# Second routing made per step of the first expert layer, in a fused attention and two-layer mixture-of-experts kernel

## The reference

```python
# layer 1: one expert a row
logits = x @ w_gate + modality_bias[modality_id]
e_idx  = argmax(logits); gate_w = softmax(logits)[e_idx]
out[mask] = gate_w * (relu(x[mask] @ w1[e]) @ w2[e])
# layer 2: two experts a row, routed by the output of layer 1
noisy = x @ w_gate + log1p(exp(x @ w_noise)) * noise
top2, top2_w = the two largest of noisy, softmax over them
out[mask] += top2_w[k] * (relu(x[mask] @ w1[e]) @ w2[e])
```

## Time and profile before

| | |
|---|---|
| median of 3 runs | 987.11 us (986.29 to 988.6) |
| the profiled execution's own time | 985.47 us |
| its span, first to last instruction | 983.7 us |
| mean granted TensorE clock | 0.967 |
| PE busy | 906.2 us, 92% |
| DVE busy | 540.5 us, 55% |
| ACT busy | 230.3 us, 23% |
| POOL busy | 349.9 us, 36% |

### The profile page before, as it was taken

How to read it: one execution, slowest core, us unless ns; L and a number is a source line. 1 busy time by engine, 2 the same in 40 slices (tenths; PEclk the granted TensorE clock), 3 DMA queues, 4 the chain that set the end, 5 groups by cost and what they waited for, 6 DMA issues and landing times.

```text
span 983.7 us, 22470 instructions
## 1 busy us (share of the span) xinstructions
PE 906.2 (92%) x7285; PEld 876.3 (89%) x7286; DVE 540.5 (55%) x968; ACT 230.3 (23%) x435; POOL 349.9 (36%) x364
## 2 busy tenths in 40 slices
PE   5999999999999999591499999999999999999995
PEld 5888887999999999591399999999999999999995
DVE  8888999784333343257663544435435454443532
ACT  2232333112011121054221222203213131221210
POOL 7333334324221313101542433423443424334232
PEclk9999999999999999895699999999999999999998
DMA  6676782219111112253253534525334443522233
GB/s 250 193 229 228 257 289 92 65 44 390 50 50 33 56 40 57 69 178 119 50 186 73 122 103 112 110 36 127 96 56 104 115 109 108 116 33 52 47 48 50
DMA packets 54594, 111.69 MB, mean 114 GB/s; under 512 B 8704, under 2 KB 35712, under 8 KB 54528
## 3 DMA queue, kind: packets, MB, share of 16 engines
q1 hardware_dynamic: 34896, 71.27, 21.7%
q0 software_dynamic: 15744, 34.70, 17.3%
q10 hardware_dynamic: 3888, 4.89, 1.4%
HBM read 84.84 MB, written 26.00 MB: 113 GB/s over the span
## 4 chain that ended last, share of the span: by engine, by line
PE 82%; DVE 12%; issue 3%; DMA 1%; DVEq 1%; ACT 1%; POOL 0%; POOLq 0%
PE ps L1660 22%; PE ps L1662 21%; PE ps L1661 21%; PE ps L1570 3%; PE ps L1530 2%; PE ps L1534 2%; PE ps L1476 2%; DVE grow L898 2%; PE ps L1499 2%; PE ps L1561 1%; DVE scores L913 1%; PE ps L1585 1%; PE ps L1597 1%; PE ps L1524 1%; DVE rest L883 1%
## 5 line engine op out<-in xcount | busy, mean ns | idle before, releaser
L1660 PE MATMUL ps<-x_hi,weights 128*128 128x256 f32 x984 | 279.1, 284 | 4.6 <-DVE x_lo L1374 2.6
L1662 PE MATMUL ps<-x_hi,weights 128*128 128x256 f32 x984 | 278.5, 283 | 0.0
L1661 PE MATMUL ps<-x_lo,weights 128*128 128x256 f32 x984 | 278.2, 283 | 0.0
L829 ACT ACTIVATE hid_hi<-ps 128x512 fp32r<-128x512 f32 x164 | 98.0, 598 | 539.7 <-PE ps L1662 533.1
L1379 DVE SCALAR_TENSOR_TENSOR hid_lo<-ps,hid_hi 128x512 fp32r<-128x512 f32 x164 | 112.8, 690 | 194.2 <-ACT hid_hi L829 172.5
L1660 PE MATMUL ps<-weights,hid_hi 128*128 (+1 forms) x616 | 214.2, 348 | 1.2 <-DVE hid_lo L1379 1.2
L1662 PE MATMUL ps<-weights,hid_lo 128*128 (+1 forms) x616 | 207.3, 336 | 0.0
L1661 PE MATMUL ps<-weights,hid_hi 128*128 (+1 forms) x616 | 207.2, 336 | 0.0
L1660 PEld LDWEIGHTS ps<-x_hi,weights 128*128 128x128 f32 x984 | 187.4, 190 | 6.6 <-issue 6.5
L1661 PEld LDWEIGHTS ps<-x_lo,weights 128*128 128x128 f32 x984 | 187.4, 190 | 0.0
L1662 PEld LDWEIGHTS ps<-x_hi,weights 128*128 128x128 f32 x984 | 187.2, 190 | 0.0
(11 more groups left out here) (281 smaller groups left out, 1064.4 us busy)
## 6 DMA issues: line engine op xcount, KB each, us to landing
stage<-in_moe_w_dram SPq DMA_DIRECT2D x18, 1536.0 KB, 8.2
kv_in<-in_kv_T_dram SPq DMA_DIRECT2D x24, 512.0 KB, 5.7
kv_in<-in_kv_T_dram SPq DMA_DIRECT2D x24, 448.0 KB, 3.4
w_in<-in_w_T_dram SPq DMA_DIRECT2D x24, 258.5 KB, 4.2
out_dram<-zeros SPq DMA_DIRECT2D x26, 192.0 KB
x_rows<-y_tok ACTq DMA_DIRECT2D x24, 192.0 KB
stage<-moe_rows SPq DMA_DIRECT2D x12, 384.0 KB, 4.2
stage<-in_moe_w_dram SPq DMA_DIRECT2D x2, 768.0 KB, 7.7
```

What stands on the lines that cost most here:

```text
L829: act.activation(hid_hi[:, 2 * q:2 * q + 2, :], h_ps[q], ACT.Relu).then_inc(s_hhi[l], 1)
L1660: pe.matmul(out_ps, hi, by_hi, start=first, stop=False)
L1661: pe.matmul(out_ps, hi, by_lo, start=False, stop=False)
L1662: return pe.matmul(out_ps, lo, by_hi, start=False, stop=final)
```

## The change

The pass between the layers is taken out. Instead:

- **Extra columns.** For each expert of layer 1 in use, PE multiplies the transposed w2 (a new input, loaded by SP with `load_w2T`) by layer 2's gate and noise weights (`expert_columns`, 24 f32 products with 16 columns); ACT and DVE split the result (`split_v`, `low_v`) into 16 columns beside w2. Down products of layer 1 are 400 wide; their last 16 columns are the row's second logits before its gate weight.
- **Row chains.** Two steps after step s, its rows are routed (`row_logits`, `row_first`, `row_second`, `row_places` on DVE; Exp, Ln, Exp on ACT; two small products on PE, `row_ranks`). DVE does the first two ahead of `hidden_low(s, 0)`. Noise and gate weight come in a row of `nz_dram`, gathered by POOL (`gather_noise`); SP writes the gate part once, after `first_gates`, which DVE does at the start of step 2.
- **Lists.** Each row's two entries (row number and weight) go to per-expert lists in DRAM, by four indirect writes of 8 bytes a row (`list_rows` on POOL).
- **Change of layers.** At step 11 POOL reads what the lists hold of expert 0 (of the first nine steps) and gathers the rows of layer 2's first two steps (`early_slots`). The rows of steps 11 and 12 are routed at the end of step 11, in step 12 and in layer 2's step 0. There DVE also makes the second layer's tables (`second_tables`). SP reads all lists back once.
- **Weights** of both layers are one array and one order of loading. moe_rows is cleared during attention, `out` right after it.

Cut to its core (order of each engine's new work):

```diff
@@ SP, start and each attention chunk
+            sp.dma_start(nz_dram[:, 0:E], noise).then_inc(s_noise, 16)
+            sp.wait_ge(s_const, 5)
+            sp.dma_start(list_dram..., list_sb[:, :, :]).then_inc(s_fill, 16)
...
+                clear_row(g)
+                if late(b, c) == 6:
+                    load_w2T(lookup(sp, first_i, 0, E - 1))
@@ SP, after attention
+            for g in range(G + TS):
+                clear(g)
+            sp.wait_ge(s_gate1, 1)
+            sp.dma_start(nz_dram[:, E:2 * E]..., gate_two[:, :, :]).then_inc(s_noise, 16)
...
+            with sp.Fori(1, E) as n:
+                with sp.If(n < runs):
+                    sp.wait_ge(s_vmm, n)
+                    load_w2T(lookup(sp, run_expert, n, E - 1))
+                    load_run(n, lookup(sp, run_expert, n, E - 1))
@@ POOL, first_layer_step
+                    if peeled and s == ONE:
+                        early_slots()
...
+                    split_next(s)
+                    rows_read(s + 2)
+                    gather(s + 3, 1 - u)
+                    if peeled and s == 2:
+                        pool.wait_ge(s_noise, 32)
+                        gather_noise(0, 0, early_src)
+                        gather_noise(1, 1, early_src)
+                    elif peeled and s == 3:
+                        list_rows(1)
+                        gather_noise(2, 0, early_src)
+                        list_rows(2)
+                        gather_noise(3, 1, src_row)
+                    elif late:
+                        list_rows(s)
+                        gather_noise(s, 2, src_row)
+                    elif not peeled or s > 3:
+                        list_rows(s - LAG + 1)
+                        gather_noise(s, 2 if peeled and s == ONE else u, src_row)
+                    scatter(s, j, u)
+                    if peeled and s == ONE:
+                        list_rows(ONE)
@@ POOL, early_slots
+                pool.wait_ge(s_listed, CUT * 2 * TS * 16)
+                # waits for the scatters of steps 0 to 10
+                pool.dma_start(early_list...).then_inc(s_earlylist, 16)
+                ...four gathers to first_rows_in, and a wait for them
@@ DVE, first_layer_step (row = (number, buffer, landed, ...) of step s - 2)
+                    if peeled and s == 2:
+                        first_gates()
+                    if peeled and s == 3:
+                        row_places(1, 0, early_src[:, 0:TS], None)
+                    if row:
+                        row_logits(...)   # waits for the noise of the row
+                        row_first(...)    # waits for ACT's Exp and Ln
                     hidden_low(s, 0)
+                    if row:
+                        row_second(row[0])
...
+                        if row:
+                            row_places(...)
+                        with dve.If(lookup(dve, v_now, s, 1) > 0):
+                            low_v(run + 1, v_ps)
...
                         split_x(s + 1, 1 - u, 1)
...
+                    if peeled and s == 2:
+                        row_logits(1, 0, 32, early_dst[:, 0:TS])
+                    if peeled and s == ONE:
+                        row_logits(ONE, ...); row_first(ONE, 0); row_second(ONE)
                     result_copy(...)
+                    if peeled and s == 2:
+                        row_first(1, 0); row_second(1)
+                    if peeled and s == ONE:
+                        row_places(ONE, ...)
@@ PE, slot_step
                     up(s, 0, run)
+                    if l == 0 and peeled and s == 3:
+                        row_ranks(1)
...
+                        with pe.If(lookup(pe, v_now, s, 1) > 0):
+                            expert_columns(..., v_ps)   # waits for load_w2T
+                    if l == 0 and late:
+                        row_ranks(s)
+                    elif l == 0 and (not peeled or s > 2):
+                        row_ranks(s - LAG + 1)          # waits for row_second
+                    elif l == 1 and peeled and s == 0:
+                        row_ranks(rows_done)
                     down_second(s, 0, run, two)
```

More of the change, by code:

```diff
@@ L96, in attention_moe_moe @@
                   small[:, at[2]:at[3]].rearrange("p (c e) -> p c e", e=2 * E)]
-        noise_sb = small[:, at[3]:at[4]].rearrange("p (g e) -> p g e", e=E)
-        with ExitStack() as early:
-            y_tok = [early.enter_context(nc.sbuf_tensor(f"y_tok{i}", [P, C], F32)) for i in range(2)]
-            with nc.sbuf_tensor("block_ones", [P, P], F32) as block_ones:
-                pass
-            sx, sy = ([early.enter_context(nc.sbuf_tensor(f"{n}0", [P, TS, CX], F32))] for n in ("sx", "sy"))
@@ L106, in attention_moe_moe @@
-        gx_hi = [sb(f"gx_hi{i}", [P, CC, P], F32R) for i in range(NGT)]
-        gx_lo = [sb(f"gx_lo{i}", [P, CC, P], F32R) for i in range(NGT)]
-        sb("gap", [P, 16])
-        gate_split = sb("gate_split", [P, CC, 4 * E], F32R)
-        both = sb("both", [4 * E, 2 * E])
+        WSZ = CC * F
+        y_tok = [sb(f"y_tok{i}", [P, C]) for i in range(2)]
+        with nc.sbuf_tensor("block_ones", [P, P], F32) as block_ones:
+            pass
+        sx, sy = [sb(f"sx{i}", [P, TS, C]) for i in range(2)], [sb("sy0", [P, TS, C])]
@@ L1425, in slot_step @@
                             with dve.If(change > 0):
-                                low_w1(l, run + 1, q)
+                                low_w1(run + 1, q)
+                        if row:
+                            row_places(row[0], row[1], row[4], row[5], peeled and s == ONE)
+                        with dve.If(lookup(dve, v_now, s, 1) > 0):
+                            low_v(run + 1, v_ps)
+                            dve.wait_ge(s_vlo, run + 2)
+                            dve.nop(nofuse=True)
+                        split_x(s + 1, 1 - u, 1)
+                        with dve.If(fresh > 0):
+                            low_w2(run + 1)
                     else:
@@ L1652, in early @@
+                    last.then_inc(s_code, 1)
                 def early(s):
```

1217 lines of the change are left out of this document (675 added, 542 removed).

## The result

The changed kernel takes 1045.72 us (median of four runs, 1043.63 to 1049.42), beside it the kernel before 986.7 (984.55 to 988.6): ratio 1.060, 95% interval 1.056 to 1.065. It is slower, as forecast, but by 59 us where 24 were forecast, and 1045.7 lies outside the range.

What follows compares the result with a forecast made beforehand. Both layers were taken as bound by TensorE's own matmuls, the second routing pass as a hole. Profiled 985.5 + 3 attention + 15.4 lateness + 6 clock = 1009.9, forecast 1010 us, slower; range 958 to 1040.

Steps and rivals of the forecast that it cites:

- four waits out of five: Five long TensorE waits forecast, of 10, 9, 9, 7 and 17 us.
- steps 5 to 9: Layer one: POOL keeps up, DVE's row chain makes each step 19.0 us, 1.4 more each, 7.0 in all.
- Step 2: Layer one: TensorE waits 10 us for the second run's transposed w2; the step takes 15.5 us more.
- columns 4.9: Layer one, 24 f32 products with 16 columns at 0.2 us each: 4.9 us on the path.
- one sum of 6: Clock term: 6 us in all for running at the 1.2 GHz level after the long waits.
- Steps 3 and 4: Layer one: late noise behind POOL's work, then DVE's row chains; step 3 takes 14.3 us more, step 4 9.4.
- Rival 2: POOL becomes the bound, list writes 1.9 us instead of 1.3, noise late in steps 4 to 11: 1030 us, chance 0.14.
- Step 10: Layer one's weight change: DVE's weight parts, row_places and splits hold TensorE; 21.2 us for 13.9, 7.3 more.
- Step 11: Layer one, two rows: TensorE waits in row_ranks(11) until 24.4, product at 24.7; the step takes 7.1 us more.
- Step 12 to layer two: Largest wait, noise behind early_slots: layer two's first product 40.3 us after step 12's start, before 97.9; 57.6 less.
- some 30 operations: DVE's second_tables with the list read make layer two's second step 3.5 us longer.
- The gap's gain: Between the layers: removing the routing pass saves 80.3 us; step 12's start to layer two took 97.9 before.

Runs made afterwards that it cites:

- w2T_first: Changed kernel with the second run's transposed w2 loaded before SyncE waits for the gate weights: 1026.4 us, ratio 1.039 to the kernel before.
- noise_first: Changed kernel with GpSimd's noise gathers moved ahead in step 2, first row's list writes and third noise gather ahead in step 3: 1022.8 us, ratio 1.035.
- best1: Changed kernel with noise_first, early_last and w2T_first edits, row chain later, early slots directly behind step 11's scatter, second_tables cut in two: 1000.2 us, ratio 1.011.
- before_writes: Kernel before with four indirect 8-byte-piece writes added to each layer-one step, read by nothing: 1027.1 us (1.039) on chip C; repeated on chip A, 993.9 (1.005).
- best1_no_lists: best1 without the list writes, so layer two works on padding rows: 979.8 us, ratio 0.990 to the kernel before.
- best2: best1 with list writes held until the first transposes of the step's middle, noise gathers behind the token gather: 985.2 us (0.997), again 981.3 (0.992).
- early_last: Changed kernel with early slots' preparation behind step 11's scatter and list writes, its noise gather ahead of all: 1032.4 us, ratio 1.043.

## Why the prediction was wrong

The side was right, the mechanism right for four waits out of five, the size wrong. The step that failed most is the account of steps 5 to 9: the list writes' effect on TensorE stood at nothing, and the row chain at 1.4 us a step; the runs show some 10 us of late completions there and 2.2 to 2.6 a step. Behind it come the columns' clock (4.9 forecast, 10.4 measured) and second_tables. Point by point:

- **Step 2, and the columns.** The wait was 8.35 (forecast 10), ended by the transposed w2's landing, as forecast. The term "columns 4.9" was mis-sized: 10.4, at clock 0.50. I had charged the clock loss to the waits in one sum of 6; here it is 5.5 for the columns and 2.1 for the down products behind them. w2T_first shows that the wait is only part of the reason: without it the columns still took 7.8. In step 0 the columns took 5.4 and then the first 14 of the 48 down products ran at half level: 11.0 in all instead of 8.65. The up products there took 1.95 more, with a wait of 2.12 for first_counts in them that I had not priced.
- **Steps 3 and 4.** Together 28.6 for 23.7. The wait in row_ranks(1) is there (9.70, at 280.51; I had the product at 260 to 268.8, with the noise in 11 us earlier: DVE got it at 275.08, since GpSimd stood 7.71 for transposes that came late with step 2, which ran 5.8 over its forecast). What I placed as a wait for noise in step 4 was a wait for the list in step 3: row_places(2) may not overwrite its entries before list_rows(1) has landed, and that is issued only at 302.83, behind the gather that waits for the middle of step 3. I had read the wait on s_listed in the diff and not run it through GpSimd's order. noise_first takes both out at once: 16 us less; it does not part them.
- **Steps 5 to 9**, the largest miss, 14.3 of the 37 us. "POOL keeps up" held. The chain's price of 1.4 a step was low: on chip A, without late completions, these steps take 19.8 to 20.1 on average, 2.2 to 2.6 more than 17.6. The other 10 or so in this execution (some 20 on chips B and C) go with completions of TensorE that come late while GpSimd sends the list writes: the prediction charged these writes only to GpSimd's own time, and put their effect on TensorE at nothing. No term or rival had it. The trace of before shows it in small, and at no cost. In its step 2, with four indirect transfers just issued, ACT starts the second quarter's half 1.15 us behind its last product instead of 0.32, and 0.41 to 0.53 in steps 4 to 9:

```profile
220.92 0.28 PE L1662 MATMUL ps<-x_hi,weights 128*128 128x256 f32 x1
...
222.07 0.60 ACT L829 ACTIVATE hid_hi<-ps 128x512 fp32r<-128x512 f32 x1 [2.36 <-PE ps L1662]
```

  Rival 2 forecast a time near the measured one (1030, by a full GpSimd), for a reason that did not happen: GpSimd is busy 63.8 of 130 us. Without these 10 us the kernel would take near 1036 (an estimate, 1045.7 less 10): inside the range, still at twice the change forecast, and that would have been luck.
- **Step 10**: 7.2 for 7.3, and by the way forecast: DVE's split of x behind row_places ends the wait at 21.4 (21.2 forecast). On chip A it is 6.5.
- **Step 11**: 10.1 for 7.1. The product of row_ranks(11) comes at 25.3 (24.7 forecast). What I had at nothing is behind it: step 12's first product stands 2.4 further on, 2.23 of it idle and ended by issue alone.
- **Step 12 to layer two**: the wait (12.13 at 513.25) let the down products start at +26.6 for a forecast of 26.3, right to 0.3. What follows is 7 longer: the down products take 2.1 more than the 9.1 forecast, at the lower clock, and the idle of 6.66 at 534.91 is ended by nothing but issue. In before this stretch lies under 80 us of other waits, where it can't be seen. The Trainium skill ("Runtime: NRT & Kernel Launch", Instruction fetch mechanics) says that a taken branch whose target is not in the window held has to fetch it before execution goes on; the profile shows four transfers of its instruction queues in those 6.7 us and five in the 9 of best1, and none from 400 to 440 in the loop. It fits; no run was made to test it.
- **Layer two, second step**: 10.8 for 3.5. I priced "some 30 operations" at the 0.205 of a link; they run from 557.29 to 569.5, with eight operations on 304 columns at 0.47 each, and one on 38 columns that takes 3.32 (L1403) and ends just behind GpSimd's split of w2 (560.80 to 564.32). The result copy and hidden halves stand behind them, and TensorE idles 5.77 us ahead of 572.06. best1, which puts those between, gives 5.3 back.
- **The gap's gain** was exact (before's 98.0 for 97.9), and attention cost 0.3, not 3, in this execution. The "some 4 us" of low clock in layer two's first step stand in "985.5 - 84" and in the rivals, but not in the sum of the forecast, which has that step 0.8 longer; it was 2.2 shorter.

By the table, the profiled execution is 37.7 us over the account (62.1 for 24.4). 10 of these are the late completions, of which the kernel before shows a trace but no price. The rest is terms of the sum: steps 0 and 2 are 10.0 over, mostly the clock in and behind the narrow products; steps 3 and 4 4.9, the list's wait; the chain in steps 5 to 9 4.3; steps 11 and 12 10.3, the idle times ended by issue and the lower clock; layer two's first three steps 6.0, second_tables above all. These are 45.5, against which stand the 6 of my clock term and the 3 for attention that did not come.

**What stays open.** That the added indirect writes bring the late completions that cost time is shown twice on chip C (before against before_writes; best1_no_lists against best1). Not shown: whether their pieces, their index or their number does it, and what makes it come and go. It may be the chip, but chip C showed it in one set and not in the next, so a state of the moment or of how a program was loaded is as open; and so is whether best2's placing avoids it or met neither.

## What to carry to other kernels

Removing a pass between two stages pays only if every delivery that replaces it is followed through the queues it stands in; here three of four late deliveries were one queue's order, and reordering that queue, with the row chain moved behind the second hidden half and the list writes beside the down products, turned 1045 to 1068 us into 981 to 985, 0.3 to 0.8% under the kernel before. Look up the granted clock over narrow matmuls and over what follows them: here they took 5.4, 7.8 and 10.4 us for the same work, and ordinary products at the lower level followed each time. Measure a kernel that sends many small indirect writes in more than one set of runs and on more than one chip.

## What the hardware showed that I had not expected

- The same program took 1027.1 us on one chip and 993.9 on another, each run within 0.6% of its set's median, where the kernel without its four small writes a step took 988.9 and 988.4. In the slow case TensorE's completions arrive 2 to 6 us behind the product instead of 0.32 (up to 7.6 in the changed kernel), and products then come up to 1.4 us apart instead of 0.12, with nothing named as the reason (below, from the changed kernel's step 6, up to 0.74).
- Over 48 records of 16-column products the granted clock was 0.66, after 1.00 before them, with TensorE busy for all of 7.8 us.
- A small operation of DVE can stand until GpSimd's split of w2 is over. Copies and products of 8 to 38 columns, 0.17 to 0.24 us elsewhere, took 3.32 us in the changed kernel (to 564.39, the split to 564.32) and 3.78 in early_last (to 473.73, the split to 473.69); in the kernel before a product on 280 columns took 3.76 beside a split of 3.5. Not every DVE operation does: in the changed kernel three of 8 and 16 columns (L1297 to L1299) took 0.17 each during the split of 488.50 to 491.95, and only the copy behind them stood until 491.98. What sets them apart no run here tests.

The products of the first point:

```profile
358.11 0.28 PE L1851 MATMUL ps<-x_lo,weights 128*128 128x256 f32 x1
358.61 0.38 PE L1852 MATMUL ps<-x_hi,weights 128*128 128x256 f32 x1 [0.23 <-issue]
...
360.08 0.28 PE L1851 MATMUL ps<-x_lo,weights 128*128 128x256 f32 x1 [0.22 <-issue]
360.82 0.56 PE L1852 MATMUL ps<-x_hi,weights 128*128 128x256 f32 x1 [0.47 <-issue]
```
